# Scores of a head pair in four 64x64 tiles of the array, value products per head

## The reference

```python
k_sum = k.reshape(B, H, nb, 32, D).max(axis=3)       # 24 blocks of 32 tokens
v_sum = v.reshape(B, H, nb, 32, D).mean(axis=3)
scores_l = scale * q @ k.T, kept where |i - j| < 16
scores_s = scale * q @ k_sum.T + log(32)
a = softmax(concat(scores_l, scores_s))
x = a @ concat(v, v_sum)
h = x @ w_in;  x = (max(h, 0) + alpha * min(h, 0)) @ w_out
h = x @ w_in2; x = (P(h) / (Q(h) + 1e-6)) @ w_out2   # P cubic, Q quadratic
```

## Time and profile before

| what | us |
|---|---|
| median of 3 runs | 640.69 |
| the profiled execution's own time | 642.14 |
| its span (first to last instruction) | 640.3 |
| PE busy | 616.4 |
| PEld busy | 585.6 |
| DVE busy | 429.9 |
| ACT busy | 330.1 |
| POOL busy | 197.3 |

### The profile page before, as it was taken

One profiled execution on the slowest core, in us unless ns is written; L12 is line 12 of the kernel. 1 busy time (PEld: TensorE's weight loads), 2 busy tenths in 40 slices (PEclk: granted clock), 3 DMA queues, 4 the chain that ended last, 5 costly groups with the idle time before them and its releaser, 6 DMA issues.

```text
span 640.3 us, 9900 instructions
## 1 busy us (share of the span) xinstructions
PE 616.4 (96%) x3504; PEld 585.6 (91%) x3504; DVE 429.9 (67%) x992; ACT 330.1 (52%) x838; POOL 197.3 (31%) x217
## 2 busy tenths in 40 slices
PE   5778999999999999999999999999999999999998
PEld 4768899999999999999999989999999999999996
DVE  3756555656565546565555589877887788887775
ACT  4677544343333433333233287666655676557654
POOL 4544993000000000000132357443344433444331
PEclk9989999999999999999999999999999999999999
DMA  8879951122112220201244410000000010001001
GB/s 169 193 150 271 274 104 24 36 61 62 35 27 49 48 46 6 49 1 31 70 132 132 131 34 1 1 1 34 16 2 0 2 50 1 1 1 50 2 0 50
DMA packets 82209, 37.55 MB, mean 59 GB/s; under 512 B 59760, under 2 KB 76144, under 8 KB 81776
## 3 DMA queue, kind: packets, MB, share of 16 engines
q1 hardware_dynamic: 82160, 36.92, 23.3%
HBM read 32.58 MB, written 3.15 MB: 56 GB/s over the span
## 4 chain that ended last, share of the span: by engine, by line
PE 88%; SPq 9%; DVE 1%; DMA 1%; issue 1%; ACT 0%
PE acc L860 14%; PE acc L858 14%; PE acc L859 14%; PE hid L858 10%; PE hid L860 10%; PE hid L859 10%; PE att L858 4%; PE att L860 4%; PE att L859 3%; SPq L255 3%; PE att L847 2%; PE att L826 2%; PE att L794 1%; PE att L833 1%; SPq L304 1%; DMA q_raw<-in_q_dram 1%
## 5 line engine op out<-in xcount | busy, mean ns | idle before, releaser
L858 PE MATMUL hid<-x_hi,w_in_hi 128*128 128x384 f32 x384 | 130.5, 340 | 2.5 <-DVE g_lo L707 1.8
L859 PE MATMUL hid<-x_lo,w_in_hi 128*128 128x384 f32 x384 | 129.2, 336 | 0.0
L860 PE MATMUL hid<-x_hi,w_in_lo 128*128 128x384 f32 x384 | 129.1, 336 | 0.0
L435 POOL TENSOR_TENSOR w_out_lo<-w_out_raw,w_out_hi 128x512 fp32r<-128x512 f32 x32 | 41.2, 1289 | 247.0 <-ACT w_out_hi L463 246.7
L858 PE MATMUL acc<-g_hi,w_out_hi 128*128 128x384 f32 x256 | 90.6, 354 | 0.0
L453 POOL TENSOR_SCALAR qpart<-habs,ab 128x384 f32<-128x384 f32 x64 | 43.9, 686 | 143.1 <-ACT poly L608 142.5
L860 PE MATMUL acc<-g_hi,w_out_lo 128*128 128x384 f32 x256 | 86.7, 339 | 0.0
L859 PE MATMUL acc<-g_lo,w_out_hi 128*128 128x384 f32 x256 | 86.5, 338 | 0.0
L463 ACT ACTIVATE g_hi<-hid 128x384 fp32r<-128x384 f32 x96 | 48.3, 503 | 62.1 <-PE acc L860 54.5
L707 DVE TENSOR_TENSOR g_lo<-hid,g_hi 128x384 fp32r<-128x384 f32 x64 | 35.5, 555 | 65.8 <-ACT g_hi L463 65.8
L858 PEld LDWEIGHTS hid<-x_hi,w_in_hi 128*128 128x128 f32 x384 | 72.2, 188 | 4.4 <-issue 2.1
(11 more groups left out here) (132 smaller groups left out, 1218.5 us busy)
## 6 DMA issues: line engine op xcount, KB each, us to landing
w_in_raw<-in_moe_w_in_dram SPq DMA_DIRECT2D x32, 256.0 KB, 4.3
w_out_raw<-in_moe_w_out_dram SPq DMA_DIRECT2D x16, 512.0 KB, 4.2
vw<-in_v_dram SPq DMA_DIRECT2D x32, 120.0 KB, 3.2
q_raw<-in_q_dram SPq DMA_DIRECT2D x32, 96.0 KB, 2.9
vs_raw<-in_v_dram SPq DMA_DIRECT2D x4, 768.0 KB, 7.2
out_dram<-out_sb SPq DMA_DIRECT2D x12, 256.0 KB, 2.0
k_raw<-in_k_dram SPq DMA_DIRECT2D x16, 104.0 KB
k_raw<-in_k_dram SPq DMA_DIRECT2D x16, 100.0 KB
```

The lines of the kernel that those rows point to most:

```text
L435: pool.tensor_tensor(w_out_lo[:, f, :], w_out_raw[:, f, :], w_out_hi[f][:, :].bitcast(F32), ALU.subtract).then_inc(pool_w_out, 1)
L858: pe.matmul(dst, lhs[0], rhs[0], start=start, stop=False)
L859: pe.matmul(dst, lhs[0], rhs[1], start=False, stop=False)
L860: return pe.matmul(dst, lhs[1], rhs[0], start=False, stop=stop)
```

## The change

In SC each unit and head gets a matmul of its own: 64 partitions (the head's features), 64 stationary query columns, 120 moving key columns. Head 0's scores go to the job's first bank, head 1's to the second; units with even numbers go to partitions 0 to 63 and odd ones to 64 to 127, so that three 128x120 pieces lie in each bank as before, and masks, exponentials and transposes keep their forms. In PV each unit and head has one matmul of 64 stationary value columns and 64 moving token columns; all results of the job lie in one bank, `[:, 0:384]`, already in the order of `x_hi`. The program places each of these matmuls by where its operands and its output lie: the array is 64 rows by 64 columns for the scores (four places) and 128 by 64 for the values (two places); every other matmul is 128 by 128. `qt` has no zeros any more and no memset; the copies to `qt`, `x_hi` and `x_lo` are one instruction each for two, four and four. There is one `pe_s` and one `pe_v` signal for each job instead of two. The mask's edges are set on half of the partitions each.

```diff
-    qt = place("qt", [P, 2, UNITS, P])
+    qt = place("qt", [P, 2, CH])
...
-            pool.memset(qt[:, :, :, :], 0.0)
...
                     act.wait_ge(pe_q, j + 1)
+                    copy(qt[:, s, :], bk[1][:, 0:CH]).then_inc(act_q, 1)
...
-                    for h in range(2):
-                        rows = slice(h * QT, (h + 1) * QT)
-                        last = copy(qt[rows, s, :, rows], bk[1][rows, 0:CH].rearrange("p (u r) -> p u r", u=UNITS))
-                    last.then_inc(act_q, 1)
...
                 elif stage == PV:
-                    for g in range(2):
-                        act.wait_ge(pe_v, 2 * j + g + 1)
...
-                        for h in range(2):
-                            rows = slice(h * QT, (h + 1) * QT)
-                            last = copy(x_hi[rows, c % 2, p, g * GU * QT:(g + 1) * GU * QT].rearrange("p (u r) -> p u r", u=GU),
-                                        bk[g][rows, 0:GU * P].rearrange("p (u r) -> p u r", u=GU)[:, :, rows])
-                        last.then_inc(act_x, 1)
+                    act.wait_ge(pe_v, j + 1)
+                    if c >= 2:
+                        act.wait_ge(pe_h, (c - 1) * FT)
+                    copy(x_hi[:, c % 2, p, :], bk[0][:, 0:CH]).then_inc(act_x, 1)
...
                 elif stage == PV:
-                    for g in range(2):
-                        dve.wait_ge(act_x, 2 * j + g + 1)
...
+                    dve.wait_ge(act_x, j + 1)
+                    dve.tensor_tensor(x_lo[:, chunk(j) % 2, p, :], bk[0][:, 0:CH], x_hi[:, chunk(j) % 2, p, :].bitcast(F32),
+                                      ALU.subtract).then_inc(dve_x, 1)
...
-                        pe.wait_ge(dve_x, 2 * before + 1)
+                        pe.wait_ge(dve_x, before + 1)
...
-                        pe.wait_ge(dve_x, 2 * before + 2)
+                        pe.wait_ge(act_pt, 2 * before + 2)
...
-                    for g in range(2):
-                        for u in range(g * GU, (g + 1) * GU):
-                            last = pe.matmul(bk[g][:, (u - g * GU) * KU:(u - g * GU + 1) * KU], qt[:, s, u, :], kt[:, s, u, :],
+                    for u in range(UNITS):
+                        for h in range(2):
+                            rows, tokens = slice(h * QT, (h + 1) * QT), slice((u % 2) * QT, (u % 2 + 1) * QT)
+                            last = pe.matmul(scores_of(bk, h, u // 2)[tokens, :], qt[rows, s, u * QT:(u + 1) * QT], kt[rows, s, u, :],
                                              start=True, stop=True)
-                        last.then_inc(pe_s, 1)
+                    last.then_inc(pe_s, 1)
...
-                    for g in range(2):
-                        pe.wait_ge(act_pt, 2 * j + g + 1)
-                        for u in range(g * GU, (g + 1) * GU):
-
-                            values = vw0[0:KU, u, heads(p), :] if first else vw[0:KU, s, u, :, :]
-                            last = pe.matmul(bk[g][:, (u - g * GU) * P:(u - g * GU + 1) * P],
-                                             values.rearrange("p h d -> p (h d)"), pt[0:KU, u, :],
+                    pe.wait_ge(act_pt, 2 * (j + 1))
+                    for u in range(UNITS):
+                        for h in range(2):
+                            rows, tokens = slice(h * QT, (h + 1) * QT), slice((u % 2) * QT, (u % 2 + 1) * QT)
+                            values = vw0[0:KU, u, 2 * p + h, :] if first else vw[0:KU, s, u, h, :]
+                            last = pe.matmul(bk[0][rows, u * QT:(u + 1) * QT], values, pt[0:KU, h * UP + u // 2, tokens],
                                              start=True, stop=True)
-                        last.then_inc(pe_v, 1)
+                    last.then_inc(pe_v, 1)
```

More of the change, by code:

```diff
@@ L36, in attention_two_mlps @@
     UNITS = CH // QT
-    GU = UNITS // 2
+    UP = UNITS // 2
     KW = QT + 2 * WINDOW
@@ L232, in stages, with pair_mask @@
             return [(c * NPAIR + f // 4, stage) for stage in slots.get((f % 4, n), [])]
-        def unit_mask(j, t):
-            return 0 if (half(j) == 0 and t == 0) else 2 if (half(j) == 1 and t == UNITS - 1) else 1
+        def pair_mask(j, n):
+            return 0 if (half(j) == 0 and n == 0) else 2 if (half(j) == 1 and n == UP - 1) else 1
         def vgroup(j):
@@ L683, in attention @@
                         dve.wait_ge(dve_rec, 2 * j + g + 1)
-                        dve.tensor_tensor(probs[:, s, us, :], bk[g][:, 0:GU * KU].rearrange("p (u k) -> p u k", u=GU),
-                                          prec[:, s, us].unsqueeze(2).broadcast_to([P, GU, KU]), ALU.mult).then_inc(dve_p, 1)
+                        dve.tensor_tensor(probs[:, s, us, :], bk[g][:, 0:UP * KU].rearrange("p (u k) -> p u k", u=UP),
+                                          prec[:, s, us].unsqueeze(2).broadcast_to([P, UP, KU]), ALU.mult).then_inc(dve_p, 1)
                 elif stage == PV:
-                    for g in range(2):
-                        dve.wait_ge(act_x, 2 * j + g + 1)
-                        for h in range(2):
-                            rows, xs = slice(h * QT, (h + 1) * QT), slice(g * GU * QT, (g + 1) * GU * QT)
-                            last = dve.tensor_tensor(x_lo[rows, chunk(j) % 2, p, xs].rearrange("p (u r) -> p u r", u=GU),
-                                                     bk[g][rows, 0:GU * P].rearrange("p (u r) -> p u r", u=GU)[:, :, rows],
-                                                     x_hi[rows, chunk(j) % 2, p, xs].bitcast(F32).rearrange("p (u r) -> p u r", u=GU),
-                                                     ALU.subtract)
-                        last.then_inc(dve_x, 1)
+                    dve.wait_ge(act_x, j + 1)
+                    dve.tensor_tensor(x_lo[:, chunk(j) % 2, p, :], bk[0][:, 0:CH], x_hi[:, chunk(j) % 2, p, :].bitcast(F32),
+                                      ALU.subtract).then_inc(dve_x, 1)
             def slot(c, f, n):
@@ L831, in attention @@
                         pe.wait_ge(dve_p, 2 * j + g + 1)
-                        for u in range(g * GU, (g + 1) * GU):
-                            last = pe.transpose(bk[g][0:KU, (u - g * GU) * P:(u - g * GU + 1) * P], probs[:, s, u, :], ident[:, :])
+                        for n in range(UP):
+                            last = pe.transpose(bk[g][0:KU, n * P:(n + 1) * P], probs[:, s, g * UP + n, :], ident[:, :])
                         last.then_inc(pe_t, 1)
@@ L872, in hidden1 @@
                 if pairs[-1] < KD - 1:
-                    pe.wait_ge(dve_x, 2 * max(pairs[-1] + 1, 2))
+                    pe.wait_ge(dve_x, max(pairs[-1] + 1, 2))
                 elif f == 0:
-                    pe.wait_ge(dve_x, 2 * NPAIR * (c + 1))
+                    pe.wait_ge(dve_x, NPAIR * (c + 1))
                 if c == 0:
@@ L911, in hidden2 @@
                 if i < 2:
-                    pe.wait_ge(dve_x, 2 * JOBS)
+                    pe.wait_ge(dve_x, JOBS)
                 elif i < 4:
```

60 lines of the change are left out of this document (30 added, 30 removed).

## The result

The kernel after takes 634.53 us (median of 4 runs, 633.36 to 634.93) against 640.67 (639.88 to 644.03, 4 runs) for the kernel before beside it: ratio 0.9891 [0.9866, 0.9915], 6.1 us less. The direction of the forecast holds, but it had only 3.3 us less. A second comparison gave 633.17 against 640.49, 0.9888 [0.9867, 0.991], 7.3 us less. The profiled execution of the kernel after took 633.36 us, with a span of 631.5 (before: 642.14 and 640.3).

The account below looks back on a forecast made before the run. PE was taken as the bound, busy without gap from 66.16 to 369 us. Eleven jobs at 0 for scores and -0.62 for values give -6.8, switches +3.5: -3.3 us, median 637.4 us, range 629 to 655.

Parts of the forecast that it names:

- The order of records (scores, 0 forecast): Scores stage on PE: a matmul's second record waits for its first, then the next starts beside it; 1.34 us, nothing gained.
- all places at once: Rival: array places stream together without any limit of order, scores -0.72 and values -0.67 us a job; 628.9 us, chance 0.12.
- The order of records (values, 0.72 forecast): Value products on PE: same order of pairs, 13 x 0.055 = 0.72 us instead of 1.34, -0.62 us a job.
- The switches: Array shape changes four times a job, 44 in all, at 0.08 us each: +3.5 us; high end 0.35 each, 15.4.
- full stop: Rival: each shape switch lets the last record run out and lays the load bare, 0.35 us; 649.3 us, chance 0.10.
- The sum: Whole kernel: 11 x (0 - 0.62) = -6.8, plus 3.5 for switches, gives -3.3 us; median 637.4 us.
- 66.16 us as a fixed point: PE's wait for job 5's keys and queries: their loads fix this time, so PE's gains before it are waited away.
- The loads in a row: Rival: streams overlap but weight loads do not, 1.33 us in either stage, switches +3.5; 644.2 us, chance 0.20.
- no places at once: Rival: the array works on one matmul at a time, scores +1.13 us a job, values 0; 656.6 us, chance 0.16.
- Other engines' copies "worth nothing": ACT's and DVE's shorter copies lie beside PE's products, gaining nothing; later signals are covered, `x_lo` by 2.5 us.

Follow-up runs that it names:

- grouped: Kernel after with each stage's matmuls ordered place by place (three per place in scores, six per head in values): 648.04 us, ratio 1.0117 to the kernel before.
- doubled: Kernel after with the twelve matmuls of each stage, scores and values, issued twice in a row: 649.83 us in one execution.
- orders: Kernel after with three score orders by turns, job by job: two of them two places at a time, one pairs at one place; 634.78 us, one execution.
- split_scores: Kernel after with four of the twelve score matmuls of jobs 5 to 15 moved earlier as a stage of their own: 637.64 us, ratio 0.9939.
- pieces: Kernel after with the copies to `qt`, `x_hi` and `x_lo` cut into pieces as before: 637.42 us against 641.72, ratio 0.9943.
- after again: The unchanged kernel after, measured again in more rounds beside its variants: 633.17 us against 640.49 for the kernel before, ratio 0.9888.
- alpha_early: Kernel after with `prelu_alpha` on its own semaphore, loaded ahead of the first weights; early use of a and b moved behind the first block: 632.67 us, ratio 0.9888.
- ab_late: Kernel after with `prelu_alpha` loaded early on its own semaphore and a and b loaded behind the values of job 3: 630.44 us against 640.49, ratio 0.9841.

## Why the prediction was off

**The order of records (scores, 0 forecast): this step failed.** The prediction put it so: "only then can the next matmul start beside the second", 13 x 0.103 = 1.34 us. The runs show instead that the second record of a matmul waits for its place while the next matmul starts at another, 7 ns later. The scores stream in 0.61 us, not 1.34: -0.72 a job and -7.9 in eleven, the very value of the case "all places at once", which had a chance of 0.12. The reason given, that all records of the trace start in program order, came from a trace where every record went to the same place. It could not speak of two. `grouped` shows that the program's order matters after all, by the rule above as an order of each place with three records waiting. The Trainium skill (TensorE: Matmul & The Clock Gate, The mechanism) holds that matmuls start and end strictly in the order of the program. The starts in `grouped` don't agree: the record at 70.426 us is by its place the seventh of the program, and the fourth starts at 70.522. With four tiles by turns, as in the kernel after, nothing of this is seen.

**The order of records (values, 0.72 forecast): right in size.** They stream in 0.70 us, 12 x 0.058. With two places and rounds of 0.058 both cases had nearly the same number (0.72 and 0.67), so this agreement said nothing for the forecast's reason.

**The switches (44 x 0.08 = 3.5 forecast): mis-sized.** A way in and out costs 0.35 us, so 22 x 0.35 = 7.7 us in all: half of the high end of 0.35 a switch. The nearest row was the earlier trace rows, 0.42 instead of 0.34, and that row has a switch of the moving width, not of the array. The Trainium skill (TensorEngine Tiling (Array Packing), Key Properties) says that a change of the mode drains TensorE. The runs agree with it in part: the loads are idle for 0.25 and 0.16 us around the stage. But the first small record starts 0.07 us before the modelled end of the last wide one (90.764 and 90.834 us), so a full stop with a bare load, as the prediction priced it, isn't seen.

**The sum.** 11 x (-0.72 - 0.64) = -15.0, +7.7, gives -7.3; measured are -7.5 in the profiled part, and -6.1 and -7.3 in the medians of the two comparisons. The two errors were -7.9 and +4.2 us, and partly hid each other: that the forecast missed by only 3 to 4 us is luck.

**The loads in a row, no places at once: both fell.** 24 loads lie in 0.62 us.

**66.16 us as a fixed point: right in effect, wrong in its cause.** The queries of job 5 start at 64.85 us, and in this execution PE waits neither for them nor for the keys, where the prediction expected a wait. SP issued those keys at 54.27 us instead of 57.83, as its timeline has it (the line below), and the wait for the small constants held PE up to 49.20. Over the kernels of this study with an unchanged start (values or scores alone, doubled, grouped, orders, split, pieces, after again) the point lies between 63.5 and 65.3 us and doesn't go with PE's work, which `doubled` has most of (65.32). `split_scores`, with no more work there than the kernel after, has 65.33. The 1.3 us between the two profiled executions are of the size of this scatter; the medians gain 6.1 and 7.3 us, no more than the part behind the point gives, so no gain in front of it can be told.

```profile
54.27 0.84 SPq L255 DMA_DIRECT2D k_raw<-in_k_dram  x2
```

**Other engines' copies "worth nothing": right for the whole change, wrong part by part.** No wait appeared on PE, but only because both edits came together. One signal a job with copies in pieces costs 2.6 us (`pieces`). The prediction looked at job 6, in the middle of a chunk, and gave `x_lo` 2.5 us of spare time; at a chunk's last job the next product needs it at once.

## What to carry to other kernels

Small matmuls at different places of the array overlapped fully here, even plain fp32 ones with two records each, as long as the program alternated places after one or two matmuls. Ordered place by place, they took longer than the wide ones they had replaced (1.735 and 1.558 us a stage instead of 1.34). Count each visit to another shape at some 0.35 us of bare PE time, so gather small matmuls in one stage instead of spreading them (a stage of scores won 0.73 us by streaming and gave half back). And judge a later signal at the tightest place of the loop, the border between two chunks, not in its middle.

## What the runs showed of the hardware

- Records at four 64x64 places start 7 ns apart; one place's follow by 0.102 us for 120 fp32 columns, 0.058 for 64.
- An idle place can stay idle while records for another are ahead in the program (`grouped`: the second place starts 0.26 us behind the first). A window of three waiting records for each place gives the lengths of all six orders within 0.02 us; it is inferred from starts, since a record doesn't carry its place.
- Going to a smaller array shape and back costs 0.35 us, for 64x64 and for 128x64 alike, with 24 or 48 records in between (and 8 and 16 for 64x64).
- Behind the wait of 3.97 us for a constant the clock was at 1.2 GHz from 48.5 to 55.3 us; behind the wait of 1.3 us in `alpha_early` and `ab_late` it stayed at 2.4 GHz, while in `grouped` it fell at 48.9 us behind a wait of 1.5 us. Without the long wait alone (`alpha_early`) the kernel was not faster by anything that can be told.
